# The last chunk's first products of units 3 to 7, in two stretches of 192 tokens in place of one of 384

## What is computed

```
kv  = einsum('bhsd,bhse->bhde', k, v)         # 4 batches, 8 heads, 576 tokens, 64
out = einsum('bhsd,bhde->bhse', q, kv);  out = out / rms(out) * g_norm
x   = out as (2304 tokens, 512)
g   = x @ w_gate;  x = (silu(g) * (x @ w_val)) @ w_out        # first mixture, inner width 1536
h   = x @ w_in;    y = (max(h, 0) + log1p(exp(-|h|))) @ w_out # second mixture, inner width 2048
```

## Time and profile before

| | us |
|---|---|
| median of three runs | 886.56 |
| the profiled execution, device time | 886.71 |
| its span, first to last instruction | 884.9 |
| TensorE matmuls busy | 876.9 (99%) |
| weight loads busy | 814.6 (92%) |
| VectorE busy | 649.9 (73%) |
| ScalarE busy | 440.5 (50%) |
| GpSimd busy | 230.0 (26%) |

### The profile page before, as it was taken

The page is one execution under the profiler, slowest core; times in us unless marked ns, Lnnn a source line. Parts: engine busy times, 40 slices in busy tenths (PEclk is TensorE's granted clock), DMA queues, the critical chain, the costliest instruction groups (busy, mean ns, idle before and its releaser), DMA issues.

```text
span 884.9 us, 14699 instructions
## 1 busy us (share of the span) xinstructions
PE 876.9 (99%) x5362; PEld 814.6 (92%) x5362; DVE 649.9 (73%) x1254; ACT 440.5 (50%) x778; POOL 230.0 (26%) x189
## 2 busy tenths in 40 slices
PE   8999999999999999999999999999999999999998
PEld 7999999999999999999999998998998999999997
DVE  3655655788585877676777998878878878878875
ACT  4627454765342534342445764544554554554553
POOL 4643203599511399630255000000000000000000
PEclk9999999999999999999999999999999999999999
DMA  9985765542100022100033110000000000000100
GB/s 274 221 209 155 158 132 134 153 128 73 37 1 1 1 72 73 46 16 1 1 118 122 48 48 0 36 0 0 36 0 0 36 0 0 36 0 0 37 1 36
DMA packets 95541, 53.93 MB, mean 61 GB/s; under 512 B 37248, under 2 KB 86528, under 8 KB 95488
## 3 DMA queue, kind: packets, MB, share of 16 engines
q1 hardware_dynamic: 95328, 53.23, 22.3%
q10 hardware_dynamic: 160, 0.00, 0.0%
HBM read 44.96 MB, written 8.26 MB: 60 GB/s over the span
## 4 chain that ended last, share of the span: by engine, by line
PE 97%; DMA 1%; issue 1%; SPq 1%; ACT 0%; DVE 0%; POOL 0%; DVEq 0%; POOLq 0%
PE bank L972 23%; PE bank L974 23%; PE bank L973 23%; PE bank L1131 8%; PE bank L1130 7%; PE bank L1129 7%; PE bank L912 1%; PE bank L905 1%; PE bank L980 1%; PE bank L878 0%; PE bank L986 0%; DMA v_rest<-in_v 0%; PE bank L867 0%; DMA q<-in_q 0%; SPq L502 0%
## 5 line engine op out<-in xcount | busy, mean ns | idle before, releaser
L972 PE MATMUL bank<-x_hi,arena 128*128 128x384 f32 x554 | 187.0, 338 | 0.0
L974 PE MATMUL bank<-x_hi,arena 128*128 128x384 f32 x554 | 186.8, 337 | 0.0
L973 PE MATMUL bank<-x_lo,arena 128*128 128x384 f32 x554 | 186.0, 336 | 0.0
L972 PE MATMUL bank<-ring,slots 128*128 128x256 f32 x504 | 142.7, 283 | 0.3 <-DVE sum_b L1616 0.3
L974 PE MATMUL bank<-ring,slots 128*128 128x256 f32 x504 | 142.6, 283 | 0.0
L973 PE MATMUL bank<-ring,slots 128*128 128x256 f32 x504 | 142.6, 283 | 0.0
L1354 ACT ACTIVATE act_a<-bank 128x384 f32<-128x384 f32 x96 | 47.2, 492 | 173.9 <-PE bank L974 173.9
L1131 PE MATMUL bank<-arena,g_lo 128*128 128x512 f32 x288 | 113.1, 393 | 0.0
L1130 PE MATMUL bank<-arena,g_hi 128*128 128x512 f32 x288 | 112.9, 392 | 0.0
L1129 PE MATMUL bank<-arena,g_hi 128*128 128x512 f32 x288 | 111.9, 388 | 0.0
L972 PEld LDWEIGHTS bank<-x_hi,arena 128*128 128x128 f32 x554 | 104.4, 188 | 4.0
(11 more groups left out here) (140 smaller groups left out, 1657.5 us busy)
## 6 DMA issues: line engine op xcount, KB each, us to landing
stage<-in_moe_w_out SPq DMA_DIRECT2D x28, 256.0 KB, 3.5
out_dram<-out_stage SPq DMA_DIRECT2D x18, 256.0 KB, 2.1
k<-in_k SPq DMA_DIRECT2D x16, 256.0 KB, 3.3
v<-in_v SPq DMA_DIRECT2D x16, 256.0 KB, 3.3
stage<-in_moe_w_in SPq DMA_DIRECT2D x16, 256.0 KB, 2.8
xy<-in_q SPq DMA_DIRECT2D x48, 72.0 KB, 3.0
stage<-in_moe_w_gate SPq DMA_DIRECT2D x12, 256.0 KB, 3.7
stage<-in_moe_w_val SPq DMA_DIRECT2D x12, 256.0 KB, 4.1
```

What stands on the lines that cost most here:

```text
L972: nc.tensor.matmul(ps, hi, rhs_hi, start=first, stop=False)
L973: nc.tensor.matmul(ps, hi, rhs_lo, start=False, stop=False)
L974: return nc.tensor.matmul(ps, lo, rhs_hi, start=False, stop=last)
```

## The change

A second form of `up2`, `up2_by_columns`, runs the 12 matmuls over tokens 0 to 191 of the chunk and then once more over tokens 192 to 383, into the two halves of the same bank. It waits for the unit's weights, as `up2` does, and once for the chunk's split data. It raises `hid_done` once, behind both stretches. It is called for units 3 to 7 of the last chunk alone; everything else is as it was, on TensorE and on the other engines.

```
+        def up2_by_columns(c, f, size):
+
+            wait_low2(pe, f)
+            pe.wait_ge(xs_ready, c * KT + (NC1 * KT + KT))
+            for o in range(0, CH, size):
+                cols = slice(o, o + size)
+                for t in range(KT):
+                    last = passes(hid_ps[f % RING2][:, cols], w2_in(f, 0, t), w2_in(f, 1, t),
+                                  x2_hi[:, t, cols], x2_lo[:, t, cols], t == 0, t == KT - 1)
+            last.then_inc(hid_done, 1)
...
         for f in range(LAG2, NF2):
-            up2(NCH - 1, f)
+            if f < NF2 // 2:
+                up2_by_columns(NCH - 1, f, CH // 2)
+            else:
+                up2(NCH - 1, f)
             down2(NCH - 1, f - LAG2)
```

## The result

Six runs of the changed kernel took 889.23 to 892.08 us, median 890.48; six of the kernel before 886.12 to 887.71, median 886.53. The ratio is 1.0041, 95% interval 1.0030 to 1.0051: slower, by 2.7 to 4.5 us. The forecast was 889.5, so the median lies 1.0 us above it and, as a number, on that of rival 1 (890.5): the time alone doesn't tell the two apart, the trace does. The profiled execution took 889.65 us with a span of 887.9 (forecast 889.65 and 887.8). That it agrees to the hundredth is luck in part: single executions scatter by some 2 us (see "The change once more").

A forecast was written before the change was run, and what follows sets the result against it. TensorE, without idle time in the last chunk, was taken as the bound: 120 pairs at 0.112 us add 13.44 us, less 10.5 us removed, +2.9 on the median of 886.56, so 889.5 us; range 888.3 to 890.9.

The forecast's parts named there:

- rival 1: Units 3 to 7: load and 12 ns foot add up to 120 ns a pair, +3.9, 890.5 us; chance 0.18.
- The bound: Last chunk: TensorE has no idle time, so every 0.1 us added between matmul starts comes out at the end.
- The reserves: Units of the last chunk: ScalarE had 2.0 us and VectorE 0.8 us a unit to spare, waiting longer after the change.
- The removed part: Units 3 to 7: 60 matmuls of 384 columns with their loads go, at 175 ns each, 10.5 us.
- The price of a pair: Units 3 to 7: each added 192-column matmul with its load costs 112 ns, 13.44 us for 120; bounds 80 and 120.
- the columns' line: Straight line through matmul times at 256, 384 and 512 columns, some 12 ns at its foot; 93 ns at 192.
- The eight attention matmuls: Attention matmuls with full loads, 0.111 us each, used as agreement with the 0.11 us load, not as proof.
- The sum: Whole kernel: 13.44 us added less 10.5 removed, +2.9 us, 889.5 us on the median.
- the matmul's foot: The some 12 ns at the foot of the columns' line, which might be paid behind the load too.
- rival 2: Units 3 to 7: columns alone set the pace, 93 ns a pair, +0.7, 887.3 us; chance 0.12.
- rival 3: Ten narrow stretches: gaps of 0.2 us each add 2.0 us to the 2.9, 891.5 us; chance 0.03.
- rival 4: Between 821 and 881 us: TensorE isn't the bound and idle time soaks up the added 2.9 us; chance 0.02.

The follow-up runs named there:

- The change once more: The changed kernel run again unaltered, against the kernel before: ratio 1.0034, interval 1.0021 to 1.0046; +2.96 us from the second mixture's first matmul to the last matmul.
- over thirteen: The change made in units 3 to 15 of the last chunk in place of 3 to 7, against the kernel before: ratio 1.0094, +7.68 us in the stretch.
- three stretches: Three stretches of 128 columns in units 3 to 7 in place of two of 192, against the kernel before: ratio 1.0123, +9.73 us in the stretch.

## Why the prediction was right

**The bound.** TensorE without idle time in the last chunk, each added 0.1 us visible at the end: right. 0.6 us a unit arrives whole at the last matmul, over five units and over thirteen. The reserves (ScalarE's 2.0 us, VectorE's 0.8) grew, as put.

**The removed part.** 60 x 175 ns = 10.5 us stands; the trace after shows units 8 to 15 at the old pace.

**The price of a pair.** 112 ns was taken between 80 and 120. Measured: (10.5 + 2.96) / 120 = 112 ns. The step that carried it, that the columns' line gives 93 ns but a load occupies its path for 0.11 us and the longer of the two decides, is confirmed from three sides: a narrower matmul doesn't lower it (128 columns), 256 columns beside it are slower by their columns, and a load of half the width brings the pace under 90, while half the weights at 384 columns change next to nothing. The lower end of 80 ns was worked out with 53 ns for 128 columns, where the rows give 54 to 55; 81 or 82 ns would have changed nothing. The eight attention matmuls had the right number; whether they are bound by loads or by their own form remains open.

**The sum.** +2.9 predicted, +2.94 at the last matmul of the profiled execution, +2.96 from the start of the second mixture. The median of the first six runs lay 1.0 us above the forecast. The range held it because it took in rival 1 and 0.4 us for scatter; 1.0 us of scatter was more than it had reckoned with. The second set of runs gives 1.0034, which is 3.0 us on 886.5; the two profiles of the change agree to 0.01 us in the stretch it can touch; and at equal granted clock the first six runs give +2.8 and +3.0. So the surplus isn't the change's. As far as the record tells, it goes with the share of runs at the lower clock; the traces show scatter ahead of the second mixture, which the change doesn't touch.

**The rivals.** 120 ns a pair (rival 1): wrong, the distance is 112, although its 890.5 us is the median that was measured; the matmul's foot isn't added behind the load. The columns alone (rival 2): wrong with full loads; with half loads they come to 88 or 89 ns. Gaps (rival 3): none. Loss soaked up (rival 4): none.

**Two figures of the Trainium skill.** Both are of its page "TensorE: Matmul & The Clock Gate". The estimate of 107 ns for a load, from the section "LDWEIGHTS (loading the stationary operand)", is 5 ns below the 112 ns measured from load to load; what the 5 ns are, no run shows. The estimate of some 89 ns for a pair at 192 columns in a steady stream, from the section "Back-to-back issue gap", isn't reached here with full loads. At the two widths for which that section gives a figure, 81 ns at 128 columns and 131 at 512, the traces have 112 ns (three stretches) and 229 ns.

**A detail not foreseen.** I expected `down2` at 2.06 us as before, and named a change of its pace as a sign of being wrong. It shows 2.09 to 2.10 behind narrow matmuls, and `up2` 2.66 and not 2.69. Their sum is as predicted and units 8 to 15 have 2.10 and 2.06 as before, so the price stands and only its place in the records was put wrong.

## What to carry to other kernels

In this kernel a matmul with 128 columns of weights of its own (type fp32r, 32 bits) takes the longer of its load (112 ns) and its columns (175 ns at 384, 120 at 256). Splitting it costs little as long as both parts keep their columns above the load, some 237 of them by the line between the rows (256 less 8 ns at 0.43 ns a column: an estimate): two matmuls of 256 columns take 240 ns by the rows where one of 512 takes 229. Below that every part cost the same 112 ns, at 192 and at 128 columns, with new weights or the same ones again. So before splitting a product for finer hand-over, count the parts and multiply by the load, and look whether the consumer waits for it at all, and for how long: here ScalarE and VectorE had time to spare before, and more after. And compare runs at the same granted clock, where the difference looked for is of the size of their scatter.

## What the runs showed of the hardware that I had not expected

The stretch of 402.21 us from the second mixture's first matmul to the kernel's last repeated to 0.01 us between two kernels on different occasions, and the 405.17 us of the change too; in these profiles the scatter, some 2 us, lies ahead of it. And the distance of matmuls isn't only the longer of two things: with weights of 64 columns, 384 columns took 173 ns in place of 175, and 192 columns 89 (from the whole: (10.52 + 0.21) / 120), below the 93 of the line drawn through full loads.
